# First expert layer: slots ahead of the next best logits, tokens ahead of the best rows, gathered rows turned one gather at a time, ranks in another order

## The reference

```python
def _moe_ref(x, w_gate, w1, w2):            # x 1536 x 512, 8 experts, F = 1024
    cap = N // E                            # 192
    logits = x @ w_gate
    order = np.argsort(-logits.flatten())
    for idx in order:                       # greedy: best logit first
        tok, e = (int(idx) // E, int(idx) % E)
        if assigned[tok] >= 0 or counts[e] >= cap:
            continue
        assigned[tok] = e
        counts[e] += 1
    for e in range(E):
        mask = assigned == e
        h = np.maximum(x[mask] @ w1[e], 0.0)
        out[mask] = h @ w2[e]
```

## Time and profile before

| | us |
|---|---|
| median of three runs | 642.2 |
| lowest and highest | 641.81 to 643.93 |
| the profiled execution's own time | 641.11 |
| its span in the profile | 639.1 |

### The profile page before, as it was taken

The page is one execution under the profiler, slowest core; times in us unless marked ns, Lnnn a source line. Parts: engine busy times, 40 slices in busy tenths (PEclk is TensorE's granted clock), DMA queues, the critical chain, the costliest instruction groups (busy, mean ns, idle before and its releaser), DMA issues.

```text
span 639.1 us, 11496 instructions
## 1 busy us (share of the span) xinstructions
PE 619.7 (97%) x4384; PEld 482.4 (75%) x4384; DVE 360.8 (56%) x1132; ACT 295.3 (46%) x539; POOL 146.8 (23%) x152
## 2 busy tenths in 40 slices
PE   6999999999999999888999999999999999999996
PEld 3767777777767766367898989898899877777773
DVE  6876777677776776886968778786512220000000
ACT  5877777777777676542525344352212111111111
POOL 5340303031322921210110101010342124333201
PEclk9999999999999999999999999999999999999999
DMA  8938836455454100272644435373897769999970
GB/s 184 240 87 187 191 80 157 99 136 125 109 186 97 51 11 1 108 278 70 222 143 147 157 132 196 118 257 110 278 358 275 271 217 326 341 367 350 333 268 20
DMA packets 73393, 116.38 MB, mean 182 GB/s; under 512 B 33799, under 2 KB 37161, under 8 KB 73058
## 3 DMA queue, kind: packets, MB, share of 16 engines
q1 hardware_dynamic: 68738, 106.75, 54.1%
q0 software_dynamic: 4016, 8.80, 4.0%
q10 hardware_dynamic: 576, 0.01, 0.0%
HBM read 87.76 MB, written 12.23 MB: 156 GB/s over the span
## 4 chain that ended last, share of the span: by engine, by line
PE 91%; DVE 4%; ACT 1%; issue 1%; DMA 1%; SPq 0%; POOL 0%; POOLq 0%; DVEq 0%
PE psB L1061 14%; PE psB L1075 13%; PE psB L353 10%; PE psB L338 9%; PE psB L1804 9%; PE psB L1819 9%; PE psA L323 7%; PE psA L325 5%; PE psB L368 2%; PE psA L997 2%; PE psB L1096 1%; PE psB L281 1%; PE psB L292 1%; PE psA L1036 1%; PE psB L1989 1%
## 5 line engine op out<-in xcount | busy, mean ns | idle before, releaser
L474 DVE TENSOR_REDUCE mx<-psA 128x1 f32<-128x768 f32 x96 | 91.8, 956 | 52.1 <-PE psA L325 50.6
L542 ACT ACTIVATE prob<-psA,ebi,esc 128x768 f32<-128x768 f32 x96 | 95.2, 992 | 23.8 <-DVE ebi L419 19.4
L1061 PE MATMUL psB<-xgT,w 128*128 128x192 f32 x512 | 91.4, 331 | 0.3 <-ACT xgT L1159 0.3
L1075 PE MATMUL psB<-hT,w 128*128 128x192 f32 x512 | 88.2, 329 | 0.0
L1061 PEld LDWEIGHTS psB<-xgT,w 128*128 128x128 f32 x512 | 82.5, 190 | 6.6 <-issue 5.9
L1075 PEld LDWEIGHTS psB<-hT,w 128*128 128x128 f32 x512 | 82.7, 190 | 0.3
L338 PE MATMUL psB<-cst,prob 128*128 128x128 f32 x576 | 78.8, 273 | 0.3
L323 PE MATMUL psA<-kH,qT 128*128 128x384 f32 x192 | 74.2, 387 | 2.8 <-ACT kB L581 1.6
L338 PEld LDWEIGHTS psB<-cst,prob 128*128 128x128 f32 x576 | 66.8, 140 | 5.3 <-DVE pT L487 1.9
L353 PE MATMUL psB<-pT,v_in 128*64 128x384 f32 x360 | 68.0, 499 | 0.0
L593 ACT COPY pT<-psB 128x512 f32<-128x512 f32 x96 | 55.9, 582 | 25.6 <-PE psB L338 25.0
(11 more groups left out here) (289 smaller groups left out, 877.8 us busy)
## 6 DMA issues: line engine op xcount, KB each, us to landing
w<-in_moe_w SPq DMA_DIRECT2D x34, 2048.0 KB
kH<-hi SPq DMA_DIRECT2D x30, 192.0 KB
q_in<-in_q SPq DMA_DIRECT2D x16, 192.0 KB, 4.1
k_in<-in_k SPq DMA_DIRECT2D x16, 192.0 KB, 4.3
v_in<-in_v SPq DMA_DIRECT2D x8, 384.0 KB, 3.6
x_scratch<-x_of_batch SPq DMA_DIRECT2D x2, 1536.0 KB, 6.8
x_scratch<-x SPq DMA_DIRECT2D x8, 384.0 KB
qT<-hi SPq DMA_DIRECT2D x15, 192.0 KB
```

Of the source, the lines that this page charges most:

```text
L474: nc.vector.tensor_reduce(mx[:, u:u + 1], psS[u % 2][:, :, 0:HALF], AX.XY, ALU.max).then_inc(s_dv, 1)
L542: nc.scalar.activation(prob[:, u % 2, :, :], psS[u % 2][:, :, 0:HALF], ACT.Exp, bias=ebi[:, u:u + 1], scale=esc[:, u:u + 1], accum_out=den ...
L1061: ins = nc.tensor.matmul(ps[:, (f % 2) * CAP:(f % 2 + 1) * CAP], w1[:, k % 2, d, f * P:(f + 1) * P], xgT[:, k % 2, d, :], start=d == 0, st ...
L1075: ins = nc.tensor.matmul(ps[:, (d % 2) * CAP:(d % 2 + 1) * CAP], w2[:, k % 2, f, d * P:(d + 1) * P], hT[:, k % 2, f, :], start=f == 0, sto ...
```

## The change

Four parts, all in the first expert layer.

1. In `best` of VectorE, `slots` comes first, directly behind the members. `full`, `M` (now lines 1250 and 1251, before at the end of `taken`) and `m` follow it, then `tokens`. The updates of `left` and `open_` leave `slots` and become the function `gone`, which runs behind `tokens`.
2. In the plan `tokens` comes ahead of `best`. In the passage from round 0 to 1 the warming matmuls are split anew: 7 ahead of places, 3 ahead of tokens, 6 ahead of best and 14 behind it, 30 as before.
3. `xt` goes by gather: item ("xt", k, i) waits for the i-th gather alone and turns all 512 columns of its 96 rows. `h` starts once both are copied.
4. `ranks` takes columns 8 to 11 first, which wait for VectorE's copy, and then 0 to 7, which wait for ScalarE's.

```diff
--- before.py
+++ after.py
@@ -701,20 +701,22 @@
 
     for r in range(ROUNDS):
 
-        some = [1, 0, 0, 8, 2, 5, 3, 1, 1, 1, 2] if r > 1 else [1, 1, 0, 4, 0, 3, 2, 1, 1, 0, 1]
+        some = [1, 0, 0, 8, 2, 5, 3, 1, 1, 1, 2] if r > 1 else [1, 0, 0, 4, 0, 3, 2, 1, 1, 0, 1]
         if r:
             idle(r - 1, 7)
             steps.append(("places", r - 1))
             fill(some[0])
+            idle(r - 1, 3)
+            steps.append(("tokens", r - 1))
+            idle(r - 1, 20 if r > 1 else 6)
+            steps.append(("best", r))
+            idle(r - 1, 14)
+            work += expert(r - 1)
         else:
             idle(r, 4)
-        steps.append(("best", r))
-        fill(some[1])
+            steps.append(("best", r))
         if r:
-            idle(r - 1, 3)
-            steps.append(("tokens", r - 1))
-            idle(r - 1, 20)
-            work += expert(r - 1)
+            fill(some[1])
         else:
             idle(r, 12)
         for n, j in enumerate(BY_ACT if r else []):
@@ -1006,13 +1008,14 @@
                 ins.then_inc(s_used, 1)
             elif st[0] == "ranks":
                 r = st[1]
-                for j in range(NJ):
+
+                for j in list(range(8, NJ)) + list(range(8)):
                     if j == 0:
                         pe.wait_ge(s_ca, r + 1)
                     if j == 8:
                         pe.wait_ge(s_cd, r + 1)
                     ins = nc.tensor.matmul(psC[:, j * E:(j + 1) * E], cT[:, j * P:(j + 1) * P], selE[:, :],
-                                           start=j == 0, stop=j == NJ - 1, skip_group_check=True)
+                                           start=j == 8, stop=j == 7, skip_group_check=True)
                 ins.then_inc(s_rk, 1)
             elif st[0] == "limit":
                 pe.wait_ge(s_cm, st[1] + 1)
@@ -1037,17 +1040,14 @@
                                                tokb[:, j:j + 1], start=j == 0, stop=j == NJ - 1)
                 ins.then_inc(s_pt, 1)
             elif st[0] == "xt":
-                _, k, half = st
+
+                _, k, i = st
+                n = 2 * k + i
                 ps = enter(pe, use[st])
-                if half == 0:
-                    for n in (2 * k, 2 * k + 1):
-                        pe.wait_ge(s_xg[n % NX], 16 * (n // NX + 1))
-                for c in range(2):
-                    for i in range(2):
-                        ins = nc.tensor.transpose(
-                            ps[:, c * CAP + i * HT:c * CAP + (i + 1) * HT],
-                            xg[0:HT, (2 * k + i) % NX, (2 * half + c) * P:(2 * half + c + 1) * P],
-                            cst[0:HT, C_ID:C_ID + HT])
+                pe.wait_ge(s_xg[n % NX], 16 * (n // NX + 1))
+                for c in range(KD):
+                    ins = nc.tensor.transpose(ps[:, c * HT:(c + 1) * HT], xg[0:HT, n % NX, c * P:(c + 1) * P],
+                                              cst[0:HT, C_ID:C_ID + HT])
                 ins.then_inc(s_f, 1)
             elif st[0] == "h":
                 _, k, f = st
@@ -1056,8 +1056,8 @@
                 if f == 0:
                     pe.wait_ge(s_w1[k % 2], 16 * (k // 2 + 1))
                 for d in range(KD):
-                    if f == 0 and d % 2 == 0:
-                        pe.wait_ge(s_e, emptied(("xt", k, d // 2)))
+                    if f == 0 and d == 0:
+                        pe.wait_ge(s_e, emptied(("xt", k, 1)))
                     ins = nc.tensor.matmul(ps[:, (f % 2) * CAP:(f % 2 + 1) * CAP],
                                            w1[:, k % 2, d, f * P:(f + 1) * P], xgT[:, k % 2, d, :],
                                            start=d == 0, stop=d == KD - 1)
@@ -1153,11 +1153,11 @@
                 act.wait_ge(s_used, 3 * (r + 1))
                 nc.scalar.copy(cT[:, 0:1024].rearrange("p (b n) -> p b n", b=2), rows2[:, :, :]).then_inc(s_ca, 1)
             elif st[0] == "xt":
-                _, k, half = st
+                _, k, i = st
                 n = use[st]
                 act.wait_ge(s_f, n + 1)
-                nc.scalar.copy(xgT[:, k % 2, 2 * half:2 * half + 2, :],
-                               psW[n % NWB][:, 0:2 * CAP].rearrange("p (c t) -> p c t", c=2)).then_inc(s_e, 1)
+                nc.scalar.copy(xgT[:, k % 2, :, i * HT:(i + 1) * HT],
+                               psW[n % NWB][:, 0:KD * HT].rearrange("p (c t) -> p c t", c=KD)).then_inc(s_e, 1)
             elif st[0] == "h" and st[2] % 2:
                 _, k, f = st
                 n = use[("h", k, f // 2)]
@@ -1223,6 +1223,8 @@
             ins = nc.vector.tensor_scalar(hit[:, j, 0:CAP], iota[:, :], sl[:, j:j + 1], None, ALU.is_equal)
         ins.then_inc(s_sl, 1)
 
+    def gone(dve, k):
+
         if k < ROUNDS:
             nc.vector.tensor_tensor(left[:, :], left[:, :], memb[:, :], ALU.subtract)
             link(dve, nc.vector.scalar_tensor_tensor(out=open_[:, :], in0=open_[:, :], scalar=atop[:, :], in1=open_[:, :],
@@ -1243,10 +1245,15 @@
             elif st[0] == "best":
                 r = st[1]
 
+                slots(dve, r - 1)
+
+                link(dve, nc.vector.tensor_scalar(full[:, :], cnt[:, :], float(CAP), -BIG, ALU.is_ge, ALU.mult))
+                link(dve, nc.vector.tensor_tensor(M[:, :, :], M[:, :, :], full[:, :].unsqueeze(1).to_broadcast(allj),
+                                                  ALU.add))
                 nc.vector.tensor_reduce(m[:, :], M[:, :, :], AX.X, ALU.max).then_inc(s_m, 1)
+                tokens(dve, r - 1)
+                gone(dve, r - 1)
                 dve.wait_ge(s_m, r)
-                slots(dve, r - 1)
-                tokens(dve, r - 1)
                 pick(nc, dve, link, M[:, :, :], tie, m[:, :], wk[:, :, :], top[:, :],
                      Ob[:, r % 2, :, 0:E], known=True).then_inc(s_O, 1)
                 dve.wait_ge(s_row, 3 * r)
@@ -1323,12 +1330,10 @@
                                                   AX.X, ALU.add))
                 if r < ROUNDS - 1:
                     members(dve, r)
-                    link(dve, nc.vector.tensor_scalar(full[:, :], cnt[:, :], float(CAP), -BIG, ALU.is_ge, ALU.mult))
-                    link(dve, nc.vector.tensor_tensor(M[:, :, :], M[:, :, :], full[:, :].unsqueeze(1).to_broadcast(allj),
-                                                      ALU.add))
             elif st[0] == "places" and st[1] >= ROUNDS - 1:
                 members(dve, st[1])
                 slots(dve, st[1])
+                gone(dve, st[1])
                 tokens(dve, st[1])
             elif st[0] == "place":
                 place(dve, *st[1:])
```

## The result

Over eight runs each the changed kernel takes 648.76 us (646.59 to 653.54), the kernel before 643.22 us (641.80 to 644.33). The ratio is 1.0103, with a 95% interval of 1.0081 to 1.0124: slower, by 5.5 us between the medians. The profiled execution of the changed kernel took 648.88 us, its span is 646.9 us, 7.8 more than the span of before.

What follows compares the result with a forecast made beforehand. TensorE, at work 97% of the time, was taken as the bound. First round -0.30, second +0.95 and four later rounds +5.64 gave +6.29 us on a 642.2 median: 648.5 us, range 646.9 to 650.2 (646.6 with rival A).

Steps and rivals of the forecast that it cites:

- Third to sixth round: Four later rounds: TensorE idles until the hits are made, y resumes later, +1.41 us each, +5.64 in all.
- P: Start of a round's places matmuls on TensorE, from which the forecast counts its times in us.
- Second round: Second round: y resumes at P + 4.83 instead of P + 3.88, +0.95 us.
- First round: First round: sooner tokens and ranks bring gathered rows and first h sooner, -0.30 us, bounds -0.57 to 0.
- TensorE: tokens at 272.45, six warming matmuls of 0.224: First round, TensorE: tokens start at 272.45 us, then six warming matmuls run until 274.41.
- rival B: New gaps of 1.36 us make the granted clock fall to 1.2 GHz: 655.3 or 689 us, chance 3%.
- The other zeros: Later rounds' xt by gather and ranks, and left and open updated behind tokens: each 0 us.
- ScalarE's Sign: First round: Sign waits for the third best-rows copy; ScalarE is free at 279.4, 0.1 us to spare before the xt copies.
- Rival A: Part of the loss is taken back later: at most 1.52 us at the layer's end, +4.8, 647.0 us, chance 8%.
- Rivals C and D: TensorE never idle, other things fill the gap: 641.9, 2%; routing chain sets the pace, sooner slots shorten rounds: 639.6, 2%.

Runs made afterwards that it cites:

- the kernel with both repairs and the wait of SyncE: Changed kernel with 12 warming matmuls before first-round tokens, two y groups there later, SyncE's third-tile weight load held until tile 1 is gathered: 641.10 us, ratio 0.9989.
- the wider gap: Changed kernel with no group of y between places and tokens from the second round on, poured later instead: 660.25 us, ratio 1.0293.

## Why the prediction was right, and where it was not

*Third to sixth round*: predicted tokens at P + 2.80, best at P + 3.47, y at P + 4.83, +1.41 each; measured 2.80, 3.46, 4.81 to 4.82, +1.34 to +1.41. That a wider gap costs its width and a filled one nothing was shown by two edits of one table, 660.25 and 642.34 us around the 648.76.

*Second round*: predicted +0.95, measured +0.95.

*First round*: predicted -0.30, of which 0.10 is ranks and lies ahead of P; measured from P, +1.04. The step that failed is "TensorE: tokens at 272.45, six warming matmuls of 0.224". The hits were on time, P + 2.82. But I had not asked what TensorE does from the end of the three warming matmuls, P + 0.9, until then: 1.95 us of nothing, the longest gap of all. I weighed the fall of the clock (rival B) for the five later gaps only, 1.36 us long by my sum and 1.20 in the trace, where it did not fall, and took the rival's chance from those. In the first round it fell, in all four profiled kernels with this gap, and in the seven with twelve warming matmuls there never. With the clock held the step is right: first h at P + 10.59 to 10.82, where I had P + 10.86 (280.51, with P 0.10 sooner at 269.65), and 11.06 before. That the late first h costs time is read from the profiles; the times of the two kernels that differ by it alone, 646.92 and 647.64, don't settle it.

*The rule of the Trainium skill*, "TensorE: Matmul & The Clock Gate", "HAM oscillation — how this bites in real kernels", that waits between bursts return the engine to half clock, spoke against the change. The trace agrees with it in the first round (1.95 us of wait, 0.50) and not in the later ones (1.20 us, 1.00). The waits in that section's example are for DMA and longer than either of these.

*The other zeros*: xt by gather 0.05 and less, ranks 0.1 as taken, gone nothing. ScalarE's Sign did not hold up the copies: in the kernel with both repairs and the wait of SyncE it starts at P + 7.02, where the sum has P + 7.05, and the copies begin 0.53 us behind the transposes, 0.56 before.

*Rival A*, time taken back later: about 0.08 us a round and 0.1 behind the rounds, 0.5 in all, and not the 1.5 it was priced at. *Rivals C and D* did not happen; TensorE waited for the hits in every round.

*The total* of 648.5 against 648.76 is closer than its parts, and that is luck: the median of before was 1.0 us above the 642.2 that I started from, and the difference 5.5 and not 6.3. The first round was 1.2 us worse than I had it, and the median difference of 5.5 us is smaller than the 7.8 of the two profiled executions, of which 0.6 lies ahead of the change. Executions of one kernel differ by as much as these terms.

## What to carry to other kernels

When a step is moved ahead of another on a bound engine, write down for each place what that engine does until the moved step's input is there; here the step that was moved back had been the filling. A wait may be harmless while work in front of it covers it, and turn up in full when the cover is moved; one repair is more work poured in front, with the new order kept. A change can also tip a race between a small transfer and a large one far behind it, even one that hardly moves in time (how it came about here is not shown), so look at the whole trace and not only at the place of the edit.

## What the runs showed of the hardware

Waits of TensorE of 1.20 us (five a run, behind 1.4 us of y) and 1.52 us (behind twenty warming matmuls) left the granted clock at 1.00. One of 1.95 us, behind three warming matmuls, brought it to 0.50 in all four profiles that have it, from just at the end of the wait to 0.26 us behind it; of 2.60 us in three of five rounds. The length of a wait alone does not decide it: in the second layer one of 2.99 us left the clock at 1.00, and one of 1.32 us was followed by a fall 0.7 us after TensorE had gone back to work (the two rows above). What decides it these runs don't show. At 0.50 the twelve best transposes took 2.61 us (303.37 to 305.98, the wider gap) where they take 1.36 (334.52 to 335.88, the changed kernel), and the clock came back after three to four us; in the second layer of two kernels (525 to 532 and 507 to 513 us) it took six to seven.

A gather of 128 rows that POOL issued 0.10 us behind a 2 MB weight load of SyncE let its transposes start 7.25 us after its issue (524.22 to 531.47). With the load held back, SyncE, which waited for the same gather, went on 3.4 us after its issue (524.78 to 528.20), in the five other such kernels 3.4 to 4.3 us. Why the three kernels with 12 warming matmuls and without the wait of SyncE all lost this race in their profiles, and the four others without it won it or nearly so, stays open. In all seven kernels with 12 warming matmuls POOL had been idle 6.0 to 7.2 us when the records came, in the six others 5.2 to 5.5, and I did not find what delays them.
